# Attention units placed between the products of the first FFN, which goes by blocks of 384 tokens

## The reference, cut to what matters

```python
# attention: batch 4, 8 heads, 768 tokens, head_dim 48
f = 1 / (1 + exp(-f_logit))
for t in range(S):
    state = f[:, :, t, :, None] * state + einsum('bhd,bhe->bhde', k[:, :, t], v[:, :, t])
    y[:, :, t] = einsum('bhd,bhde->bhe', q[:, :, t], state)
x = y.transpose(0, 2, 1, 3).reshape(3072, 384)        # tokens x (head, dim)
x = ((x @ w_a) * (x @ w_b)) @ w_out                    # first FFN, 384 -> 1536 -> 384
p = domain_probs / (domain_probs.sum(-1) + 1e-9)       # second FFN, 4 experts, 384 -> 1024 -> 384
out = sum_e p[:, e] * (relu(x @ w1[e]) @ w2[e])
```

## Time and profile before

| | us |
|---|---|
| median of 3 runs (lowest, highest) | 1508.8 (1508.2, 1509.43) |
| span of the profiled execution | 1506.1 |
| attention stage, to the first FFN matmul | 246.5 |
| first FFN, to the second matmul group `up_2(1)` | 453.2 |
| rest of the second FFN, to its last matmul | 803.2 |

### The profile page before, as it was taken

How to read it: one execution, slowest core, us unless ns; L and a number is a source line. 1 busy time by engine, 2 the same in 40 slices (tenths; PEclk the granted TensorE clock), 3 DMA queues, 4 the chain that set the end, 5 groups by cost and what they waited for, 6 DMA issues and landing times.

```text
span 1506.1 us, 18161 instructions
## 1 busy us (share of the span) xinstructions
PE 1493.7 (99%) x7249; PEld 1259.1 (84%) x7249; DVE 437.8 (29%) x872; ACT 385.0 (26%) x681; POOL 282.6 (19%) x219
## 2 busy tenths in 40 slices
PE   7999999999999999999999999999999999999999
PEld 6666667888888888888999999999999999999998
DVE  7656652222222222222222222222222222222222
ACT  4443432322222222223211132211221112211111
POOL 5343342401010101002311141111221111411110
PEclk6555556999999999999999999999999999999999
DMA  6455532300000000001100020000110000100001
GB/s 144 109 112 119 125 78 63 95 1 22 0 1 0 0 1 1 1 1 32 53 1 0 1 64 21 1 0 1 32 53 1 0 1 0 43 22 22 22 21 43
DMA packets 39203, 49.20 MB, mean 33 GB/s; under 512 B 3792, under 2 KB 34000, under 8 KB 39120
## 3 DMA queue, kind: packets, MB, share of 16 engines
q1 hardware_dynamic: 39120, 48.04, 12.3%
HBM read 38.58 MB, written 4.72 MB: 29 GB/s over the span
## 4 chain that ended last, share of the span: by engine, by line
PE 98%; DVE 0%; issue 0%; DVEq 0%
PE bank L962 19%; PE bank L960 19%; PE bank L961 19%; PE bank L1037 9%; PE bank L1036 9%; PE bank L1035 9%; PE bank L923 4%; PE bank L918 3%; PE bank L888 3%; PE bank L900 3%; PE bank L875 1%; DVE ostage L849 0%; DVE st L725 0%; DVEq L66 0%; DVE unit L673 0%
## 5 line engine op out<-in xcount | busy, mean ns | idle before, releaser
L857 DVE SCALAR_TENSOR_TENSOR h_lo<-bank,h_hi 128x512 fp32r<-128x512 f32 x192 | 132.9, 692 | 600.9 <-ACT h_hi L558 600.9
L558 ACT ACTIVATE h_hi<-bank 128x512 fp32r<-128x512 f32 x192 | 115.1, 599 | 627.1 <-PE bank L962 627.0
L597 POOL TENSOR_TENSOR xs_lo<-xt,xs_hi 128x512 fp32r<-128x512 f32 x90 | 114.4, 1297 | 792.9 <-ACT xs_hi L491 792.9
L1037 PE MATMUL bank<-slot_hi,h_lo 128*128 128x384 f32 x768 | 259.4, 338 | 0.0
L1035 PE MATMUL bank<-slot_hi,h_hi 128*128 128x384 f32 x768 | 259.1, 337 | 0.0
L1036 PE MATMUL bank<-slot_lo,h_hi 128*128 128x384 f32 x768 | 259.1, 337 | 0.0
L962 PE MATMUL bank<-xs_lo,slot_hi 128*128 128x512 f32 x576 | 227.2, 394 | 0.0
L961 PE MATMUL bank<-xs_hi,slot_lo 128*128 128x512 f32 x576 | 226.7, 394 | 0.0
L960 PE MATMUL bank<-xs_hi,slot_hi 128*128 128x512 f32 x576 | 226.2, 393 | 0.0
L960 PE MATMUL bank<-xs_hi,wab_hi 128*128 128x512 f32 x432 | 170.3, 394 | 0.0
L961 PE MATMUL bank<-xs_hi,wab_lo 128*128 128x512 f32 x432 | 170.1, 394 | 0.0
(11 more groups left out here) (77 smaller groups left out, 1580.6 us busy)
## 6 DMA issues: line engine op xcount, KB each, us to landing
unit<-fkq SPq DMA_DIRECT2D x62, 216.0 KB, 4.1
raw<-w SPq DMA_DIRECT2D x64, 192.0 KB, 2.6
v_in<-v_chunks SPq DMA_DIRECT2D x16, 288.0 KB, 4.6
out<-ostage SPq DMA_DIRECT2D x24, 192.0 KB, 1.9
xt<-ystage SPq DMA_DIRECT2D x24, 144.0 KB, 4.2
raw<-wa SPq DMA_DIRECT2D x6, 384.0 KB, 4.0
raw<-wb SPq DMA_DIRECT2D x6, 384.0 KB, 3.8
raw<-wo SPq DMA_DIRECT2D x6, 384.0 KB, 3.1
```

Source lines behind the costliest of these rows:

```text
L558: eng.activation(h_hi[:, j % 2, :], ps_up[j % 4][:, :], ACT.Relu).then_inc(s_hhi, 1)
L597: return eng.tensor_tensor(xs_lo[g % 2][:, k, :], x_source(g)[:, k, :], xs_hi[g % 2][:, k, :].bitcast(f32), ALU.subtract)
L857: eng.scalar_tensor_tensor(out=h_lo[:, j % 2, :], in0=ps_up[j % 4][:, :], scalar=0.0, in1=h_hi[:, j % 2, :].bitcast(f32), op0=ALU.max, op1 ...
L1037: mm = eng.matmul(o, hl, w_hi, start=False, stop=(f == FT2 - 1))
```

## The change

The first FFN goes by blocks of 384 tokens (`TB1`): 8 blocks of 12, 96 steps. Its work is cut in 288 parts `j`: `up_1(i, 0)` (w_a), `up_1(i, 1)` (w_b) and `down_1(i-1)`, 9 matmuls of 384 columns each. One bank each holds a and b, three hold the block's result. The other three banks are one set for attention.

Attention keeps its unit. The units are now ordered so that four pairs (the eight heads of a batch entry) do their first 384 tokens and then their second: four units make one block of the FFN. The first six units come ahead of the FFN, three parts apart, with a second set of three banks (those of the block's result). Units 6 to 31 come every six parts, from part 2 to part 152. The list `J` holds the part at which a unit's `turn` stands; every engine's work for it has a fixed distance to it: `scores` +1, `kv` +2, `output` +5, and so on. `SPLIT_AT` puts the weight pieces at parts: seven from J[0]-6 = -24 on, two parts apart. States are kept in `st_carry` (between units) and `st_in`; `dec` and `krt` have one buffer, the ring of units four (six at the start), v is loaded per unit. The three matmuls of `three`, the arithmetic of a unit and the second FFN are as before.

```diff
+    TB1 = UT
+    NB1 = T // TB1
+    N1 = NB1 * FT1
...
+    FIRST = 6
+    RING = 4
+    VRING = 4
+    PACE, APART = 6, 3
+    START = -3 * APART * 10 // 3
+    J = [APART * (u - FIRST) for u in range(FIRST)] + [PACE * (u - FIRST) + 2 for u in range(FIRST, NU)]
+    UNIT_AT = {j: u for u, j in enumerate(J)}
+    BEGIN = J[0] - 10
...
+    def split_at(r):
+        if r < R0:
+            return J[0] - 6 + 2 * r
+        if r < R1:
+            return 2 * (r - R0)
+        return CMIN_AT + 20 + 6 * (r - R1)
...
+    def x_at(n, k):
+        return -1 if n == 0 else 36 * (n - 1) + 20 + 2 * k
...
-        ps_krt, ps_kv, ps_y, ps_att = bank[0], bank[1], bank[2:4], bank[4:8]
-        ps_out = bank[0:4]
-        ps_up = bank[4:8]
+        SETS = (bank[5:8], bank[0:3])
+        ps_out1, ps_a, ps_b = bank[0:3], bank[3], bank[4]
+        ps_out, ps_up = bank[0:4], bank[4:8]
...
 # ACT: the loop over i is now one over the parts
+            for j in range(BEGIN, 3 * N1):
+                i, part = j // 3, j % 3
+                if j >= 0:
+                    if part == 0 and i >= 1:
+                        h_round(i - 1)
+                        if i % FT1 == 1 and i > FT1:
+                            y_out(i // FT1 - 1)
+                    if part == 1:
+                        a_out(i)
+                if (u := at(j, 1)) is not None:
+                    evac_krt(u)
+                if (u := at(j, 6)) is not None:
+                    evac_y(u)
+                if (u := at(j, -6)) is not None:
+                    decays(u)
+                if (u := at(j, -9)) is not None:
+                    logs(u)
+                if j in SPLIT_AT:
+                    split_hi(SPLIT_AT[j])
...
 # POOL
+                if (u := at(j, -5)) is not None:
+                    gates(u)
+                if j in SPLIT_AT:
+                    split_lo(SPLIT_AT[j])
...
 # DVE: gate, h_rest and y_out_1 of the FFN at their parts, then
+                if (u := at(j, 2)) is not None:
+                    mask(u)
+                if (u := at(j, 3)) is not None:
+                    state(u)
+                if (u := at(j, -5)) is not None:
+                    ends(u)
+                if (u := at(j, -3)) is not None:
+                    keys(u)
...
 # TensorE
-            up_1(0)
-            for i in range(N1):
-                up_1(i + 1) if i + 1 < N1 else up_2(0)
-                down_1(i)
+            for j in range(BEGIN, 3 * N1):
+                i, part = j // 3, j % 3
+                if j >= 0:
+                    if part < 2:
+                        up_1(i, part)
+                    elif i >= 1:
+                        down_1(i - 1)
+                if (u := at(j, 0)) is not None:
+                    turn(u)
+                if (u := at(j, 1)) is not None:
+                    scores(u)
+                if (u := at(j, 5)) is not None:
+                    output(u)
+                if (u := at(j, 2)) is not None:
+                    kv(u)
...
+            down_1(N1 - 1)
+            up_2(0)
```

More of the change, by code:

```diff
@@ L284, in x_source, with x1_ready, x1_free, x2_source @@
+        X_DONE = []
+        x_all = [0, 0]
+        for u in range(NU):
+            x_all[u % 2] += 16 * len(list(x_parts(u)))
+            X_DONE.append(x_all[u % 2])
+        def x1_ready(eng, n):
+            last = PPB * (n + 1) - 1
+            eng.wait_ge(s_x[last % 2], X_DONE[last])
+            eng.wait_ge(s_x[(last - 1) % 2], X_DONE[last - 1])
+        def x1_free(eng, n):
+            if n >= 2:
+                eng.wait_ge(s_upb, FT1 * (n - 1))
+        def x2_source(g):
             b = g % NB
@@ new lines, in x2_hi, with a_out, h_round @@
+            def x2_hi(g):
+                x2_ready(eng, g)
+                x2_free(eng, g)
+                for k in range(KT):
+                    eng.activation(xs_hi[g % 2][:, k, :], x2_source(g)[:, k, :], ACT.Copy).then_inc(s_xhi, 1)
+            def a_out(i):
+                eng.wait_ge(s_upa, i + 1)
+                if i >= 1:
+                    eng.wait_ge(s_h, i)
+                eng.activation(a_sb[:, :], ps_a[:, 0:TB1], ACT.Copy).then_inc(s_a, 1)
+            def h_round(i):
+                eng.wait_ge(s_h, i + 1)
+                if i >= 2:
+                    eng.wait_ge(s_down, i - 1)
+                eng.activation(h_hi[:, i % 2, 0:TB1], h_sb[:, :], ACT.Copy).then_inc(s_hhi, 1)
@@ L581, in decays, with gates @@
-            def decays(u):
+            for u in range(3, FIRST):
+                eng.memset(unit_ring[u][0:64, :, :], 0.0).then_inc(s_pad2, 1)
+            def gates(u):
+                n = ring(u)
                 eng.wait_ge(s_inv, u + 1)
-                if u == 0:
-                    eng.wait_ge(s_in[0], 32)
-                k = unit[0:P2, u % RING, K, :]
-                eng.tensor_tensor(k, k, unit[0:P2, u % RING, F, :], ALU.mult).then_inc(s_kg, 1)
+                eng.wait_ge(s_in[n], 32 * loads_in_ring(u))
+                k = unit_ring[n][0:P2, K, :]
+                eng.tensor_tensor(k, k, unit_ring[n][0:P2, F, :], ALU.mult).then_inc(s_kg, 1)
@@ L914, in output @@
                     t = slice(cc * CH, (cc + 1) * CH)
-                    o = ps_y[u % 2]
-                    if c > 0:
-                        eng.matmul(o[0:P2, t], st[0:P2, g % SLOTS_ST, :], unit[0:P2, u % RING, Q, t], start=True, stop=False,
-                                   skip_group_check=True)
-                    for n, first in enumerate((0, 64)):
+                    begins = half_of(u) == 0 and cc == 0
+                    if not begins:
+                        eng.matmul(o[0:P2, t], st_before(u, cc)[0:P2, :], unit_ring[ring(u)][0:P2, Q, t], start=True,
+                                   stop=False, skip_group_check=True)
@@ L926, in output @@
                 mm.then_inc(s_y, 1)
-            eng.wait_ge(s_const, 2)
-            for n in range(WARM_UP):
-                eng.matmul(ps_att[0][:, 0:128], ident[:, :], ident[:, :], start=True, stop=True)
-            eng.wait_ge(s_set, 5)
-            for i in range(NU + 2):
-                if i < NU:
-                    turn(i)
-                    scores(i)
-                if 1 <= i <= NU:
-                    kv(i - 1)
-                if i == NU:
-                    eng.wait_ge(s_min, 2)
-                    eng.wait_ge(s_krt, NU)
-                    eng.transpose(ps_krt[0:1, 0:P2], cmin[0:P2, :], ident[0:P2, 0:P2]).then_inc(s_mint, 1)
-                if i >= 2:
-                    output(i - 2)
@@ new lines, in _ @@
+            for n in range(WARM_UP):
+                eng.matmul(bank[3][:, 0:128], ident[:, :], ident[:, :], start=True, stop=True)
+            eng.wait_ge(s_set, 5)
+            for j in range(BEGIN, 3 * N1):
+                i, part = j // 3, j % 3
+                if j >= 0:
+                    if part < 2:
[10 more added lines that the diff above has]
+                    kv(u)
+                if j == CMIN_AT:
+                    eng.wait_ge(s_min, 2)
+                    eng.wait_ge(s_st, states(NU, 0))
+                    eng.transpose(bank[5][0:1, 0:P2], cmin[0:P2, 0:1], ident[0:P2, 0:P2]).then_inc(s_mint, 1)
```

915 lines of the change are left out of this document (475 added, 440 removed).

## The result

The changed kernel takes 1440.5 us (median of 4, 1439.7 to 1442.6), against 1508.8 us before: a ratio of 0.9554, 95% interval 0.9536 to 0.9573. The forecast was 1445 (1428 to 1495).

What follows compares the result with a forecast made beforehand. Attention was taken as bound by TensorE's own queue at half clock. Terms 66.5 + 454.7 + 96.2 + 10.4 + 3.9 + 1 + 1 + 805.3 + 3.2 = 1442.2 us of span; median 2.7 over, so 1445 (1428 to 1495).

Steps and rivals of the forecast that it cites:

- the hand-over: From down_1(95) to the second FFN: 1 us of TensorE waiting, as down_1(94) gives only 1.6 us of cover.
- Pace of the first FFN: First FFN: 2592 matmuls of 384 columns at 0.1754 us, 454.7 us; smaller blocks cost 3.6 us.
- Attention at full clock: Units 6 to 31 between FFN groups: 3.7 us each instead of 7.12, 96.2 us for 26.
- its returns: First FFN matmul behind each attention piece: about 0.1 us extra, four a unit, 10.4 us in all (0 to 18).
- The part ahead: Six units before the first FFN matmul, at half clock with first turn at 19.5: 66.5 us (57.6 to 76).
- Half clock at the start of the FFN: Start of the FFN: output(5) still at half clock, 3.9 us, and first FFN matmuls 1 us over full pace.
- Waits: Mixed stage with single banks and buffers: waits on other engines covered by FFN matmuls, costed at nothing.
- Second FFN: Second FFN: same instructions as before, 803.2 us plus 2.1 for up_2(0), 805.3 us.
- the clock fell nowhere in the mixed stage: Rival, mixed stage: clock does not hold between pieces; 1534 us if only attention runs at half clock; chance 0.14.
- the waits that were feared: Rival, mainly first block: late weight pieces or scans hold up TensorE through in-order lists, +20 to +50, 1465 to 1495; chance 0.20.
- a unit kept 4.3 us, not 6.2: Rival, mixed stage: issue, not clock, bounds attention's pieces, about 6.2 us a unit, 65 more, 1510 us; chance 0.04.

Runs made afterwards that it cites:

- the run with fillers on the kernel before: Kernel before, with eight identity matmuls (float32, 128x128) added to each of the attention units: 1468.0 us, ratio to before 0.9735.
- later splits: Changed kernel with the first seven weight pieces split at parts -13 to -1 instead of -24 to -12: 1432.6 us, ratio to before 0.9492.
- the run with fillers in front of it: Changed kernel, first seven splits later, w_out's behind block 0's input roundings, plus 14 float32 matmuls between down_1(95) and the branch: 1434.3 us.
- the thinned FFN: Changed kernel with one of the three matmuls of each first-FFN product, three between attention pieces instead of nine: 1200.3 us, measured once, result not the reference's.
- fillers in ten units only: Kernel before with the identity matmuls added in units 0 to 9 and none in units 10 to 31: 1492.9 us, ratio 0.9887.
- all units ahead: Changed kernel with all 32 attention units ahead of the first FFN matmul, everything else kept: 1561.9 us, ratio to before 1.0352.
- block 0's input first: Changed kernel, first six splits moved later, w_out's split behind the roundings of block 0's input, pieces from the eighth three parts later: 1428.8 us, ratio 0.9469.
- with fillers at either end: Changed kernel, splits later and w_out's behind block 0's input roundings, plus identity matmuls ahead of the first FFN (1429.1 us) or 14 matmuls before the second (1434.3 us).
- later splits with fillers in the part ahead: Changed kernel with the first seven splits at parts -13 to -1, identity matmuls between pieces ahead of the FFN and 40 warm-up matmuls: 1433.3 us, ratio 0.9515.
- a unit every nine parts: Changed kernel with an attention unit every nine FFN parts instead of six, 81 FFN matmuls between units instead of 54: 1440.3 us, ratio 0.9558.

## Why the prediction was right

The sum was 1442.2 us of span, the profile has 1438.3. The mechanism was right; that the sum came so near is in part luck. From the first FFN matmul to the second FFN it had 567.2 us and the profile 567.9, but by errors that cancel: the FFN's pace and `output(5)` were put too high by 5.5 and 1.7 us, the units and the hand-over too low by 5.2 and 2.5. The 5.1 us gained in the second FFN were not foreseen at all. To come from span to median it added 2.7 us; in the profiled execution itself the difference is 1.8 (1440.07 and 1438.3). Step by step:

1. *Pace of the first FFN.* Forecast 0.1754 us a matmul, 454.7. In the stretch without attention, 500 to 600 us, 577 start in 100 us: 0.1733, so 449.2 for 2592. Over by 5.5 us. The estimate came from the second FFN of before, where they stand among 512-column ones.

2. *Attention at full clock.* Forecast 3.7 a unit and 0.4 for its returns. The two kinds of unit have 4.12 and 4.34 for both; 12 of the 26 are of the first kind and 14 of the second, 110.2 us. Over the stage: 567.9 less 449.2, less 2.2 for `output(5)`, 1.2 for FFN matmuls at half clock and 3.5 at the hand-over leaves 111.8, 4.3 a unit, against 106.6 forecast for 26, 5% more. No row of before shows attention's pieces at full clock, and the rows of the warm-up have PEclk 1.00 at both paces, 0.200 and 0.103 us; that their ratio is the clock's was my estimate. It was nearly right: the run with fillers on the kernel before has 3.8 a unit at a clock of 1.00 against 7.12 at 0.50, 0.54 for 0.52.

3. *The part ahead.* Forecast 66.5, measured 66.89. Its inside was less exact: the first `turn` came at 21.0, not 19.5, the copy of `krt` at 29.5 (forecast 29), `kv(0)` at 29.96 (forecast 29.3). DVE's `keys` took 1.33 us, with POOL at work beside it, where it was put at 0.6; the next unit's took 0.54. One later wait, 1.35 us for DVE's states ahead of `output(1)`, was not foreseen, and was made up by units that took 6.7 to 6.9 us, a little under my 6.95. The runs with later splits confirm the cause: without it the part ahead is 11 to 12 us shorter.

4. *Half clock at the start of the FFN.* `output(5)` was put at half clock, 3.9 us; the clock rose at 69.7, ahead of it (0.50 from 68 to 69 us, 0.62 from 69 to 70, 1.00 from 70 to 71), so it took about 2.2.

5. *Waits.* None inside the mixed stage, as forecast: the view of waits shows TensorE waiting there for nothing but 0.33 us at the hand-over. There I had 1 us; it was 0.33 for DVE and 2.99 without a releaser, 3.5 with the slower first matmuls, so this term was too small by 2.5 us. TensorE's list has a branch between `down_1(95)` and `up_2(0)` (the general form, which is not taken); before, the branch stood between attention and the first FFN and showed no gap. That it stood behind attention's slow matmuls there is not the reason: in the run with fillers in every unit attention ends at full clock, and the first FFN matmul (206.98) follows the last of `output` (206.63) with no idle time either. What the branch skips differs as well: 2 matmuls in the kernel before, 650 in the changed one. That the branch is the cause is argued from its place and from the run with fillers in front of it; no run took it away, made the skipped part shorter or moved it.

6. *Second FFN.* Forecast 805.3 as before, measured 800.2 and 5 under, for a reason that stays open.

The rivals: the clock fell nowhere in the mixed stage, the waits that were feared did not come, and a unit kept 4.3 us, not 6.2. The mixed stage has a clock of 1.00 with TensorE busy for 564.59 of 567.90 us and no idle time between its groups; in the thinned FFN, where TensorE does idle, dips to 0.63, 0.66 and 0.86 do show. That TensorE is busy was not enough here for the full clock: in the profile of before, attention's small float32 matmuls kept it busy for all of the 200 us from 40 to 240 at 0.50, and the same queue with eight identity matmuls a unit ran at 1.00. The few quicker executions of before are a reminder that what decides between the two is not fully known.

## What to carry to other kernels

A busy TensorE at a granted clock of 0.50 was here a resource that other work unlocked: look at PEclk beside the busy share, and where small matmuls fill the queue at half clock, try dense ones between them, real ones if there are any. The small ones went from 7.12 to 3.8 us a unit with the identity matmuls between them, and to 4.3, returns included, with the FFN's. With either, the clock stayed at 1.00 as long as the dense ones kept coming; with fillers in ten units only, it did so for some seven microseconds longer in the profiled execution. Look at the mean clock of every execution, not of the profiled one alone. When lists of several engines are merged by a table of positions, the start deserves its own look: the weight splits placed ahead of the first units' work cost 8 us, where all the waits of the steady stage came to nothing.

## What the runs showed of the hardware that was not expected

- Eight identity matmuls a unit, 128x128 float32, added to a stage that TensorE bounds, made the kernel 2.7% faster (0.9735).
- The full clock outlasted the last filler by some seven microseconds of attention's own matmuls with 1.65 us of idle time among them, and then went to 0.50; two other executions of that kernel had 22 to 25 us less at half clock (mean clock 0.952 and 0.953, not 0.945).
- Six of 76 executions of the kernel before (its two forms with wider tiles or a smaller scratch among them) took 1482.6 to 1503.5 us instead of about 1509, at a mean granted clock of 0.926 to 0.946 instead of 0.922: by an estimate from the mean clock it was up for part of an attention stage that had nothing added to it.
- With 2.4 to 3.4 us of idle time ahead of the second FFN the clock fell to 0.50 in five profiles (all units ahead, where it fell about 1 us behind the second FFN's first matmul; later splits; block 0's input first, and with fillers at either end; in the thinned FFN, too, with 4.0 us), and stayed at 1.00 in three others (the changed kernel, later splits with fillers in the part ahead, a unit every nine parts), with 3.0 to 3.3 us there: its length alone doesn't decide it. Executions of one and the same kernel lie 2 to 3 us apart with it (later splits: 1430.5 at a mean clock of 0.983, 1433.5 at 0.981).
- The same second FFN runs at 505 to 506 matmuls per 100 us in the programs of the changed form and 502 to 503 in those of before's (0.6%), whatever comes ahead of it.
